# The opening of a fused gated-linear-attention and feed-forward kernel: last token answered from decayed keys, and an order of its own for the first period

## What is computed

```python
f = sigmoid(f_logit)                          # B=4, H=8 heads, S=768 tokens, D=48
for t in range(S):                            # per batch and head, state is D x D
    state = f[t][:, None] * state + outer(k[t], v[t])
    y[t] = q[t] @ state
x = y as (B*S, H*D) = (3072, 384)
h = x @ w_in;  g = where(h > 0, h, exp(min(h, 0)) - 1);  x = g @ w_out     # 384 -> 2048 -> 384
h = relu(x @ w2_in);  out = (h * h) @ w2_out                               # the same sizes
```

## Time and profile before

| | |
|---|---|
| median of 3 runs | 1006.78 us (1005.01 to 1008.18) |
| the profiled execution's own time | 1007.56 us |
| its span, first to last instruction | 1005.6 us |
| PE busy | 962.6 us, 96% |
| DVE busy | 538.2 us, 54% |
| ACT busy | 391.9 us, 39% |
| POOL busy | 295.7 us, 29% |
| chain that ended last | PE 87%, DVE 6%, issue 3%, ACT 2% |

### The profile page before, as it was taken

The page is one execution under the profiler, slowest core; times in us unless marked ns, Lnnn a source line. Parts: engine busy times, 40 slices in busy tenths (PEclk is TensorE's granted clock), DMA queues, the critical chain, the costliest instruction groups (busy, mean ns, idle before and its releaser), DMA issues.

```text
span 1005.6 us, 25907 instructions
## 1 busy us (share of the span) xinstructions
PE 962.6 (96%) x11076; PEld 824.0 (82%) x11076; DVE 538.2 (54%) x763; ACT 391.9 (39%) x704; POOL 295.7 (29%) x240
## 2 busy tenths in 40 slices
PE   5758979999999999999999999999999999999998
PEld 4656868888888888888787878999999999999997
DVE  6666787867777686766425663333333333333332
ACT  2424445534443453444444443232242332422322
POOL 4446474635344363535323542000000000000000
PEclk9959999999999999999999999999999999999999
DMA  7241343130222123020003332000010010010000
GB/s 248 90 123 49 103 124 108 43 99 24 79 76 58 55 78 101 23 59 33 18 13 125 99 86 72 1 32 32 1 63 0 16 47 0 31 31 0 32 1 31
DMA packets 47236, 57.95 MB, mean 58 GB/s; under 512 B 7968, under 2 KB 39456, under 8 KB 47136
## 3 DMA queue, kind: packets, MB, share of 16 engines
q1 hardware_dynamic: 44448, 45.63, 15.1%
q10 hardware_dynamic: 2688, 10.85, 3.0%
HBM read 42.30 MB, written 9.44 MB: 51 GB/s over the span
## 4 chain that ended last, share of the span: by engine, by line
PE 87%; DVE 6%; issue 3%; ACT 2%; DMA 1%; POOL 0%; SPq 0%; DVEq 0%; ACTq 0%; POOLq 0%
PE ps L1288 8%; PE ps L1287 8%; PE ps L1292 8%; PE ps L1326 7%; PE ps L1325 7%; PE ps L1329 7%; PE ps L866 6%; PE ps L991 5%; PE ps L1012 5%; PE ps L993 5%; PE ps L998 5%; PE ps L1014 5%; PE ps L1018 5%; PE ps L917 1%; PE ps L882 1%
## 5 line engine op out<-in xcount | busy, mean ns | idle before, releaser
L1241 DVE TENSOR_TENSOR g<-g 128x512 f32<-128x512 f32 x96 | 67.1, 699 | 264.0 <-ACT g L1161 264.0
L576 POOL TENSOR_TENSOR glo<-g,ghi 128x512 fp32r<-128x512 f32 x80 | 109.4, 1367 | 236.0 <-ACT ghi L436 236.0
L1161 ACT ACTIVATE g<-ps 128x512 f32<-128x512 f32 x112 | 67.1, 599 | 284.7 <-PE ps L1292 280.4
L1287 PE MATMUL ps<-xhi,wts 128*128 128x512 f32 x336 | 131.9, 393 | 0.7 <-ACT xhi L421 0.7
L1288 PE MATMUL ps<-xhi,wts 128*128 128x512 f32 x336 | 131.9, 393 | 0.0
L1326 PE MATMUL ps<-wts,ghi 128*128 128x384 f32 x380 | 128.9, 339 | 0.0
L1325 PE MATMUL ps<-wts,ghi 128*128 128x384 f32 x380 | 127.6, 336 | 0.0
L866 PEld LDWEIGHTS ps<-q,k 48*62 48x62 f32 (+6 forms) x4992 | 83.1, 146 | 47.1 <-issue 41.3
L866 PE MATMUL ps<-q,k 48*62 48x32 f32 (+6 forms) x4992 | 90.1, 229 | 29.7 <-issue 17.1
L429 ACT ACTIVATE e<-ps 128x512 f32<-128x512 f32 x80 | 47.8, 598 | 138.7 <-PE ps L998 138.5
L991 PE MATMUL ps<-xhi,wts 128*128 128x512 f32 x240 | 99.3, 414 | 0.6 <-POOL wts L569 0.6
(11 more groups left out here) (109 smaller groups left out, 1651.5 us busy)
## 6 DMA issues: line engine op xcount, KB each, us to landing
raw<-w SPq DMA_DIRECT2D x64, 192.0 KB, 2.4
q<-qk SPq DMA_DIRECT2D x24, 256.0 KB, 4.6
gate<-fl SPq DMA_DIRECT2D x11, 512.0 KB, 4.0
k<-qk SPq DMA_DIRECT2D x11, 512.0 KB, 3.7
v<-vn SPq DMA_DIRECT2D x12, 384.0 KB, 4.4
x<-xo ACTq DMA_DIRECT2D x6, 768.0 KB, 3.3
xs<-x ACTq DMA_DIRECT2D x6, 768.0 KB, 4.3
out<-PT SPq DMA_DIRECT2D x24, 192.0 KB, 1.9
```

Source lines behind the costliest of these rows:

```text
L576: nc.gpsimd.tensor_tensor(out=glo[:, f % 2, :], in0=g[:, f % 2, :], in1=ghi[:, f % 2, :].bitcast(F32), op=ALU.subtract).then_inc(s_glo, 1)
L1287: nc.tensor.matmul(h, w(0, k), xhi[:, k, :], start=(k == 0), stop=False)
```

## The change

Eight things are done together.

1. Units 0 and 1 no longer wait for their new state to answer the last token. After level 6, `last_scores_of` multiplies the decayed keys with q of the last token (32 products of one column), `take7` copies the scores, and `last_values` multiplies them with v (32 products of one column), after `values`.
2. Transposes, `krow_copy`, `new_state` and `state_update` of these units come behind values and, on ScalarE, behind the issue of its part of the gather. GpSimd's copies of their last q fall away.
3. ScalarE's queue issues 6 of unit 1's 10 pieces instead of 5. SP's queue issues 4 pieces, a load of k, 6 pieces and 4 pieces.
4. The first loads go in another order on the two queues, and v, the gates of chunk 1 and the first weights wait each for a level product of unit 1.
5. Gates of (1, 1) and the Exp of one column are made between `take5` and `take6` of unit 1. Gates of (1, 2) and (1, 3) are made by Sigmoid as well, in the periods, and VectorE's additions and reciprocals for them fall away.
6. VectorE makes the low part of every w1 piece, GpSimd of none.
7. Only level 0 of unit (1, 0) stands ahead of the first period, which is written out on its own: hidden(1, 0) comes first, and levels 1 to 6 of (1, 0) and 0 to 3 of (1, 1) follow between hiddens and outputs.
8. In it, `transpose_keys`, `q_state`, `new_state` and `values` stand behind hidden(1, 6), and `krow_copy` behind `high(1, 6)`.

```diff
@@ SP @@
-        load_q(0, 0)
-        load_gates(0, 1)
-        load_q(0, 1)
-        load_k(0, 1)
-        sp.dma_start(ident[:], ident_d).then_inc(s_const, 16)
-        load_v(0, 0)
-        load_v(0, 1)
-        load_weights(range(FIRST_SPLIT))
-        load_gates(1, 0)
-        load_gates(1, 1)
-        load_q(1, 0)
-        load_k(1, 0)
-        load_q(1, 1)
-        load_k(1, 1)
-        gather(0, 0)
-        gather(0, 1, range(4))
+        load_q(0, 0)
+        load_q(0, 1)
+        sp.dma_start(mask_words, mask_d).then_inc(s_mask_in, 16)
+        sp.dma_start(ident[:], ident_d).then_inc(s_ident, 16)
+        sp.wait_ge(*level(s_mm, 0, 1, 0))
+        load_v(0, 0)
+        sp.wait_ge(*level(s_mm, 0, 1, 1))
+        load_gates(1, 0)
+        sp.wait_ge(*level(s_mm, 0, 1, 2))
+        load_v(0, 1)
+        sp.wait_ge(*level(s_mm, 0, 1, 3))
+        load_gates(1, 1)
...
+        load_q(1, 0)
+        gather(0, 0, range(3))
+        load_k(1, 0)
+        gather(0, 0, range(3, H))
+        gather(0, 1, range(3))
@@ ACT, before the periods @@
         take5(0, 1)
+        gates(1, 1, True)
+        nc.scalar.activation(warm[:, 1:2], warm[:, 0:1], ACT.Exp)
         take6(0, 0)
         take6(0, 1)
-        krow_copy(0, 0)
-        krow_copy(0, 1)
+        take7(0)
+        take7(1)
+        split_weights(range(2))
         y_copy(0, 0)
...
-        for to, at in moves(0, 1, range(4, H)):
+        for to, at in moves(0, 1, range(3, H)):
             act.dma_start(to, at).then_inc(s_x, 16)
+        krow_copy(0, 0)
+        krow_copy(0, 1)
@@ ACT, end of first_period (new) @@
+            hidden_copies(1, 4)
+            high(1, 4)
+            split_weights(split_at(1, 4))
+            take5(1, 0)
+            hidden_copies(1, 5)
+            high(1, 5)
+            split_weights(split_at(1, 5))
+            take6(1, 0)
+            gates(1, 2, True)
+            hidden_copies(1, 6)
+            high(1, 6)
+            split_weights(split_at(1, 6))
+            krow_copy(1, 0)
+            split_weights(split_at(1, 7))
+            y_copy(1, 0)
+            last_copy(1, 0)
@@ DVE, first_period (new) @@
+            x_split(1)
+            step(1, 0, 1)
+            activate(1, 0)
+            split_weights(split_at(1, 0))
+            step(1, 0, 2)
+            activate(1, 1)
...
+            step(1, 0, 4)
+            step(1, 1, 0)
+            activate(1, 3)
+            split_weights(split_at(1, 3))
+            step(1, 0, 5)
+            step(1, 1, 1)
+            activate(1, 4)
+            split_weights(split_at(1, 4))
+            step(1, 0, 6)
+            step(1, 1, 2)
+            activate(1, 5)
+            split_weights(split_at(1, 5))
+            step(1, 1, 3)
+            activate(1, 6)
@@ PE, first_period (new); feed's even slots are outputs, its odd ones hiddens @@
+            feed(1, 0, (1,))
+            product(1, 0, 1)
+            feed(1, 0, (3,))
+            product(1, 0, 2)
+            feed(1, 0, (4, 5))
+            product(1, 0, 3)
+            feed(1, 0, (6, 7))
+            product(1, 0, 4)
+            product(1, 1, 0)
+            feed(1, 0, (8, 9))
+            product(1, 0, 5)
+            product(1, 1, 1)
+            feed(1, 0, (10, 11))
+            product(1, 0, 6)
+            product(1, 1, 2)
+            feed(1, 0, (12, 13))
+            product(1, 1, 3)
+            transpose_keys(1, 0)
+            feed(1, 0, (14,))
+            q_state(1, 0)
+            new_state(1, 0)
+            values(1, 0)
+            feed(1, 0, (15,))
+            last_column(1, 0)
@@ PE, before the periods @@
+        last_scores_of(0)
+        last_scores_of(1)
+        values(0, 0)
+        last_values(0)
+        values(0, 1)
+        last_values(1)
         transpose_keys(0, 0)
         transpose_keys(0, 1)
         new_state(0, 0)
-        values(0, 0)
         new_state(0, 1)
-        last_column(0, 0)
-        values(0, 1)
-        last_column(0, 1)
-        for l in range(EARLY):
-            product(1, 0, l)
+        product(1, 0, 0)
+        first_period()
+        period(1, 1)
```

More of the change, by code:

```diff
@@ L183, in krow @@
     def krow(c, h):
-        return xo[:, 0:UB, :] if second(c, h) else krow_all[:, :, :]
+        if not past(c, h, 2):
+            return xo[:, 0:UB, :] if h else e[:, :, :]
+        return krow_all[:, :, :]
     def ys(c, h):
@@ L509, in _ @@
                 .to_broadcast([HP, MASKED, X, 32]), ACT.Copy).then_inc(s_mask, 1)
-        split_weights(range(2))
         take4(0, 0)
@@ L525, in _ @@
         act.wait_ge(s_lasty, 2)
-        for to, at in moves(0, 1, range(4, H)):
+        for to, at in moves(0, 1, range(3, H)):
             act.dma_start(to, at).then_inc(s_x, 16)
+        krow_copy(0, 0)
+        krow_copy(0, 1)
         split_weights(range(2, FIRST_SPLIT))
-        gates(1, 1, True)
-        nc.scalar.activation(warm[:, 1:2], warm[:, 0:1], ACT.Exp)
-        for c in range(1, NC):
+        first_period()
+        period(1, 1)
+        for c in range(2, NC):
             for h in range(2):
@@ L626, in _ @@
             k_update(0, 1, l)
-        split_weights(range(2))
         keep_last(1, 0)
-        for l in range(2):
-            k_update(1, 0, l)
-        split_weights(range(2, FIRST_SPLIT))
-        for l in range(2, EARLY):
-            k_update(1, 0, l)
-        for c in range(1, NC):
+        k_update(1, 0, 0)
+        k_update(1, 0, 1)
+        first_period()
+        period(1, 1)
+        for c in range(2, NC):
             for h in range(2):
@@ L765, in period @@
             split_weights(split_at(c, f + 3))
-            if more(c, h, 2):
+            if c > 1 and more(c, h, 2):
                 denominators(c, h + 2)
@@ L803, in _ @@
         step(1, 0, 0)
-        step(1, 0, 1)
         split_weights(range(2, FIRST_SPLIT))
-        step(1, 0, 2)
-        step(1, 0, 3)
-        for c in range(1, NC):
+        first_period()
+        period(1, 1)
+        for c in range(2, NC):
             for h in range(2):
@@ L909, in values @@
             pe.wait_ge(s_ev6, count(c, h, 1, 1))
-            pe.wait_ge(s_krow, count(c, h, 1, 1))
+            if not fresh:
+                pe.wait_ge(s_krow, count(c, h, 1, 1))
             def within(u, i, par, j, half, start=False, stop=False):
```

149 lines of the change are left out of this document (99 added, 50 removed).

## The result

The changed kernel is slower: 1016.03 us (median of 5, 1012.4 to 1017.9) against 1005.42 us, a ratio of 1.0092 with a 95% interval of 1.0064 to 1.012. I had forecast 1003.2 and a range up to 1010. The profiled execution has a span of 1015.3 us (1005.6 before).

What follows compares the result with a forecast made beforehand. PE, busy 96% of the span, was taken as the bound. First period -0.1, second period -4.5 and slow clock +1.0 sum to -3.6 us, from 1006.8 to 1003.2 us; range 996 to 1010.

Steps and rivals of the forecast that it cites:

- Which sign: Whole kernel: 3.6 us faster; chance 0.50 for faster by over 0.3%, 0.32 within, 0.18 slower.
- five pairs of low parts: VectorE, first period: five pairs at 0.93 and 0.52 us, 7.3 us in all.
- `hidden(1, 0)` at 60.2: Opening: x ready and hidden(1, 0) starting at 60.2 us instead of 72.17, 12 us earlier.
- the forecast's 41.4: Opening, ScalarE: first take6 done at 41.4 us, after take5 at 38.3, Sigmoid, table load and Exp; values follow.
- VectorE's rounds: First period, level 1's end to g of block 5: VectorE's work in a row takes 38.4 us.
- The tail: First period's end: ScalarE needs 10.1 us from g(5) to krow, two table loads of 1.28 included.
- the wait for level 6: First period: PE idles about 6 us before level 6 of (1, 0), which waits for take5.
- that before q_state: First period's tail: PE waits 3.8 us before q_state, behind krow_copy.
- The second period: Second period: 2.6 of 7.1 us lost to idling and half clock remain, a gain of 4.5 us.
- The new wait for q: Start of the second period: PE newly idles 2.0 us, since load_q(1, 2) waits for values(1, 0).
- The one that ended on the slow side: Rival: clock falls at level 6 of (1, 0) and stays down, 1012.8 us; 0.18, shared with another tail wait.

Runs made afterwards that it cites:

- gather_first: The base with SP's load of k for (1, 0) behind its part of the gather instead of inside it: 1015.85 us, ratio 1.0103.
- the base: The changed kernel with the even low parts of w1 on GpSimd again, starting point of further edits: 1013.43 us, ratio 1.0069.
- tail_early: The base with krow_copy(1, 0) right behind take6 and the Sigmoid gates of (1, 2) behind the last high part: 1017.17 us, ratio 1.0100.
- old_period: The base with levels 1 to 3 of (1, 0) ahead again and the first period in its old order: 1013.91 us, ratio 1.0070.
- old_period_krow_first: old_period with krow_copy of units 0 and 1 ahead of ScalarE's part of the gather: 1009.48 us, ratio 1.0027.
- krow_first: The base with krow_copy of units 0 and 1 ahead of ScalarE's part of the gather: 1012.18 us, ratio 1.0062.
- after_again: The changed kernel run and profiled once more, no edit: 1015.54 us, ratio 1.0094 to the kernel before.
- before_low_vector: The kernel before with all low parts of w1 on VectorE, that part of the change alone: 1010.54 us, ratio 1.0046.
- after_low_gpsimd: The same kernel as the base: the changed kernel with even low parts of w1 on GpSimd again, 1013.43 us, ratio 1.0069.
- take5_early: The base with ScalarE's take5(1, 0) ahead of high(1, 4) and its two high parts: 1012.66 us, ratio 1.0061.

## Why the prediction was wrong

**Which sign.** It said 3.6 us faster with 0.50 for faster; the kernel is some 10 us slower, 6 us beyond the range. Three steps failed. The sum has no term for level 0 of (1, 0), which the new opening puts 7 to 8 us later. It has VectorE's five pairs of low parts at 7.3 us, and they took 11.6. And it lets x be ready as if TensorE's new products and SP's wait inside the gather cost nothing. The gain of the second period, a fourth, was 4.5 in the sum and 0.5 to 2.7 in the two profiles.

**`hidden(1, 0)` at 60.2: wrong by 2.75 us, and so was the mechanism.** ScalarE's take5 ended at 37.22 instead of 39.79, so the start gained 2.6 us where I had put 1.5; the direction was right. Then I took TensorE's durations from rows at full clock and let the scores of the last tokens lie beside ScalarE's work. They took 3.6 us (128 matmul records of 28 ns for the two units, L1061), against 0.54 us for the 32 records of an old last column. ScalarE had the first take6 done at 40.43, and values waited for the scores until 41.39. That is the forecast's 41.4, by luck: 1.1 us of better start against 1.0 of scores that were not covered. Values of unit 0 took 3.1 us instead of 1.9, and last_values 1.4 instead of 0.5, so SP's gather started at 46.21 and not at 44.6. ScalarE's y copy of unit 0 still started earlier than before, but SP then stood from 49.62 to 52.27 at `load_k(1, 0)`, which waits for the transposes, and these now stand behind values of both units. I had put that wait at nothing. In gather_first, without this stall and with the load behind it, x was ready 4.4 us earlier; 1.1 of that was there when the gather began (45.29 against 46.43 in the base), and it did not pay alone.

**What I left out of the sum: level 0 of (1, 0).** The forecast gives it no time; it starts `hidden(1, 0)` when x is there. Level 0 started at 59.7, behind both units' values, transposes, ScalarE's six issues (5.18 us, from 50.67 to 55.85; I had them from 47 to 52) and krow_copy. In tail_early's profile the transposes ended at 51.57, and the next product still waited 4.96 us for krow_copy, so it is ScalarE's issues that hold level 0 there. Its step on VectorE then stood ahead of the xlo pieces, for which `hidden(1, 0)` waited 1.3 us, and all levels behind it moved. old_period and old_period_krow_first show its price with the old order of the period: 8.4 us in the medians for 7 us of delay, and 4.4 us back for 2.5. In the new order the same edit, krow_first, gave back 1.2 us, inside the intervals, since x is next.

**VectorE's rounds: the order right, the size wrong by 3.9 us.** The term is "five pairs of low parts, 0.93 and 0.52, 7.3". The five took 1.80, 2.72, 2.67, 2.67 and 1.78, or 11.6 us. That is the difference of the row, 4.3 against 3.9 (12.6 us for the five in after_again, with a row of 42.3 again). before_low_vector shows the cost in time, 5 us in the kernel before; in the changed kernel after_low_gpsimd gave back 2.1 to 2.6.

**The tail: right.** Krow came 9.95 us behind g(5), forecast 10.1; the wait for level 6 was 6.3 (forecast 6), that before q_state 3.2 (forecast 3.8). ScalarE: Activation LUTs of the Trainium skill adds a drain of 1.38 us to a table load; here exp starts at 118.64, 0.01 us behind the load from 117.35, and no gap is seen at the Sigmoid either. The measurement decides for 1.28. What these waits are worth I could not have said from the sum: take5_early took away the longest one (3.93 us in its base) for nothing that can be measured, tail_early took away the second and lost time.

**The second period: 4.5 us forecast, 0.5 had (2.7 in after_again's profile).** The wait of 3.09 us at 150.7 is still there at 160.84, with 2.72: GpSimd's k_update of (2, 0) is no longer late, but VectorE's q_update is, behind a pair of low parts of 2.67. The half-clock stretch behind it stayed too. The new wait for q was 0.8 us, with 0.4 ahead of level 4; I had 2.0.

**The rivals.** The one that ended on the slow side named the clock at level 6, with 1012.8. Half clock came with that wait, as expected (0.50 from 103.1 to 113.3 us, the wait from 100.9 to 107.2), but the wait is not what decides, since removing it gave less than 1 us. That the kernel is slower does not confirm this rival. I named no case in which the opening delays the levels, and old_period shows that this alone makes a kernel as slow as the base.

**How the loss is made up, as far as the runs show.** The opening: 8.4 us in the medians, with the old order of the period. The low parts: 5.1 us in the kernel before, 2.1 to 2.6 in the changed one. The period's new order: in the base it starts `hidden(1, 0)` 17.4 us before old_period does (62.95 and 80.37) and gives all but 1.3 us of it back by exp 15; with the tail and q's load mended it is 4.4 us ahead of old_period in the medians. These overlap and don't add up to a sum.

## What to carry to other kernels

Work taken out of a chain does not gain if the chain that starts behind it is put off: before an order is changed, write down when each later chain's first instruction can start, not only the one that the change is for. A wait of TensorE is worth removing only together with the one that stands behind it; here one edit lost 4 us alone and won 4 with the second. Work moved between VectorE and GpSimd should be priced at the other engine's whole instruction in between, and a big reordering is best tried by its parts: one small part (first loads) and one small idea of it (a hidden in a gap of the level chain) made the faster kernel.

## What the runs showed of the hardware

TensorE ran at half clock much longer at the start than I had thought, and not equally long in each profile. take5_early's profile has the granted clock from the start, and shows 0.50 from 9.3 to 53.7 us, in which TensorE was busy 80% of the time:

```profile
core 0: us, PE busy (x) PEld busy (x) DVE busy (x) ACT busy (x) POOL busy (x), PEclk, DMA share, GB/s
...
9.30:53.70 44.40, 35.67 (x1168) 33.23 (x1168) 25.38 (x33) 17.22 (x31) 20.82 (x16) 0.50 0.38 107
```

Two other profiles of kernels with the changed opening, krow_first and old_period, show 0.50 until 53.8 us. The profile of the changed kernel has no granted clock before 75.7 us and prints 1.00 there; the durations tell otherwise: matmuls of `hidden(1, 0)` at 62.95 take 0.63 us, as at half clock, and those at 78 take 0.39. In the kernel before, values of unit 0 ran at full rate at 44.01 (0.67 us for 32 records; 1.08 at 41.39 here). By the same reading the six variants of the kernel before ran them at full rate too (0.66 or 0.67 us, at 41.9 to 44.7).

With the changed opening the rise scatters, though TensorE's order up to the values is the same. gather_first rises first, between these two rows:

```profile
42.89 1.10 PE L1033 MATMUL ps<-PT,v 64*48 64x64 f32 x32
...
44.82 0.67 PE L1033 MATMUL ps<-PT,v 64*48 64x64 f32 x32
```

tail_early rises between 47.6 and 49.6, three profiles show 53.7 or 53.8, after_again rises between 65 and 68 us, and the changed kernel, the same code, at 75.7. So the order of the work does not settle it alone; what does stays open. The late rise makes values and transposes longer. What it costs at the end was not isolated: the two profiles of the changed kernel differ by 2.9 us at exp 15, the later rise being the slower one, and that is all that the runs show.
